# Fused attention and two MLPs on one core: the down-sampled attention units interleaved with the last local ones

## What is computed

```python
q_d = q.reshape(B, H, Sd, factor, D).mean(axis=3)      # factor 4: 576 -> 144 positions
k_d = k.reshape(B, H, Sd, factor, D).mean(axis=3)
v_d = v.reshape(B, H, Sd, factor, D).mean(axis=3)
out_up = np.repeat(sm_attn(q_d, k_d, v_d), factor, axis=2)
mask = np.abs(pos[:, None] - pos[None, :]) < factor     # local: 3 keys to either side
scores = np.where(mask, scale * np.matmul(q, k.transpose(0, 1, 3, 2)), -1000000000.0)
out_local = softmax(scores) @ v
x = out_up + out_local                                  # then (2304, 512)
x = (silu(rms_norm(x) @ w_gate) * (rms_norm(x) @ w_val)) @ w_out    # d_ff 1536
y = np.square(np.maximum(x @ w_in, 0)) @ w_out2                     # d_ff 2048
```

## Time and profile before

| | us |
|---|---|
| median of 3 runs (lowest, highest) | 1017.39 (1017.31, 1018.33) |
| the profiled execution, device time | 1024.89 |
| span of its trace | 1022.9 |

### The profile page before, as it was taken

The page is one execution under the profiler, slowest core; times in us unless marked ns, Lnnn a source line. Parts: engine busy times, 40 slices in busy tenths (PEclk is TensorE's granted clock), DMA queues, the critical chain, the costliest instruction groups (busy, mean ns, idle before and its releaser), DMA issues.

```text
span 1022.9 us, 16131 instructions
## 1 busy us (share of the span) xinstructions
PE 989.4 (97%) x6404; PEld 918.7 (90%) x6404; DVE 423.8 (41%) x783; ACT 322.0 (31%) x698; POOL 162.9 (16%) x151
## 2 busy tenths in 40 slices
PE   6899959999999999999999999999999999999998
PEld 5677748999999999999999999999999999999997
DVE  6678892543443443443442322323333233332322
ACT  3556554442122122122123333223222222232221
POOL 3356556640000000000002661000000000000000
PEclk9779878999999999999999999999999999999999
DMA  9968302310000000000002440000000000000000
GB/s 241 175 149 211 89 2 93 123 53 1 1 1 1 1 1 1 1 1 1 1 1 64 133 133 2 1 1 32 1 31 1 1 31 1 16 16 1 31 1 31
DMA packets 27972, 42.84 MB, mean 42 GB/s; under 512 B 2300, under 2 KB 14972, under 8 KB 27516
## 3 DMA queue, kind: packets, MB, share of 16 engines
q1 hardware_dynamic: 26316, 40.64, 14.7%
q10 hardware_dynamic: 1584, 1.18, 0.4%
HBM read 37.10 MB, written 4.72 MB: 41 GB/s over the span
## 4 chain that ended last, share of the span: by engine, by line
PE 90%; DVE 5%; issue 3%; DMA 1%; ACT 1%; POOL 1%; SPq 0%; DVEq 0%; ACTq 0%
PE bank L986 49%; PE bank L1085 20%; PE bank L1017 15%; PE bank L922 1%; PE bank L941 1%; PE bank L962 1%; PE bank L916 1%; DVE sml L683 1%; PE bank L937 1%; PE bank L973 1%; DVE mxl L662 1%; DMA kp<-k_dram 1%; DVE qd L705 1%; PE bank L911 0%; PE bank L885 0%
## 5 line engine op out<-in xcount | busy, mean ns | idle before, releaser
L986 PE MATMUL bank<-xs,wsplitB 128*128 128x384 f32 x2376 | 436.8, 335 | 0.0
L986 PEld LDWEIGHTS bank<-xs,wsplitB 128*128 128x128 f32 x2376 | 416.8, 188 | 6.9
L1085 PE MATMUL bank<-wsplitB 128*128 128x512 f32 x702 | 174.4, 393 | 0.0
L1085 PEld LDWEIGHTS bank<-wsplitB 128*128 128x128 f32 x702 | 130.7, 188 | 23.7
L840 DVE TENSOR_TENSOR prod<-sig 128x384 f32<-128x384 f32 x96 | 53.6, 558 | 222.2 <-ACT sig L605 222.2
L1017 PE MATMUL bank<-hb,wsplitB 128*128 128x384 f32 x720 | 136.1, 336 | 1.4 <-ACT hb L545 1.4
L1017 PEld LDWEIGHTS bank<-hb,wsplitB 128*128 128x128 f32 x720 | 125.6, 188 | 3.3 <-POOL wsplitB L419 1.6
L798 DVE TENSOR_TENSOR prod<-prod,bank 128x384 f32<-128x384 f32 x72 | 39.9, 554 | 192.5 <-PE bank L986 192.4
L605 ACT ACTIVATE sig<-bank 128x384 f32<-128x384 f32 x96 | 47.2, 492 | 229.5 <-PE bank L986 229.5
L545 ACT CAST hb<-prod 128x384 fp32r<-128x384 f32 x72 | 37.0, 514 | 248.1 <-DVE prod L798 248.1
L986 PE MATMUL bank<-xs,wsplitA 128*128 128x384 f32 x504 | 96.4, 343 | 3.8 <-DVE xs L766 3.8
(11 more groups left out here) (75 smaller groups left out, 746.4 us busy)
## 6 DMA issues: line engine op xcount, KB each, us to landing
wrawB<-w_dram SPq DMA_DIRECT2D x56, 256.0 KB, 3.0
vquad<-v_dram SPq DMA_DIRECT2D x16, 288.0 KB
out_dram<-work SPq DMA_DIRECT2D x18, 256.0 KB, 2.0
kp<-k_dram SPq DMA_DIRECT2D x3, 1152.0 KB, 13.7
qs<-q_dram SPq DMA_DIRECT2D x3, 1152.0 KB, 20.8
vwin<-v_dram SPq DMA_DIRECT2D x6, 512.0 KB
wrawA<-w_dram SPq DMA_DIRECT2D x12, 256.0 KB, 4.7
vwin<-v_dram SPq DMA_DIRECT2D x2, 320.0 KB
```

The costliest lines, as they stand in the source:

```text
L986: last = mm(bank[:, 0:cols], wslot(n)[:, pw, 128 * k:128 * k + 128], x[:, px, k, 0:cols], start=(i == 0 and k == 0), stop=(i == 2 and k == ...
L1085: last = mm(OUT[par][tt][:, :], gs[:, px, 128 * tt:128 * tt + 128], w[:, pw, :], start=(m == 0 and i == 0), stop=(m == J2 - 1 and i == 2))
```

## The change

The order of the units in a group becomes a string, `LLLLLLDLDLDLD` (L local, D down-sampled): six local units, then down-sampled and local ones in turn. The numbering helpers follow it. The lists of slots change with it, and so do three waits: each down-sampled unit waits only for the sums of four of its own pair of heads; the loads of the next groups wait for the last local unit, now at place 11 in the group and not at 8; the additions on GpSimd stand in four slots running.

```diff
+ORDER = "LLLLLLDLDLDLD"
+LAST_LOCAL = ORDER.rindex("L")
...
-SUM_FOUR_AT = (1, 3, 5, 7)
+SUM_FOUR_AT = (1, 2, 4, 5)
 FIRST_SUM_FOUR_AT = (4, 5, 6, 7)
-SUM_V_AT = (10, 11, 12)
-ADD_DOWN_AT = (5, 7, 11, 12)
+SUM_V_AT = (7, 8, 9)
+ADD_DOWN_AT = (5, 6, 7, 8)
...
         def local(g):
-            return g % NU < NL
+            return ORDER[g % NU] == "L"
...
-                    sp.wait_ge(qk_done, NU * (b - 2) + NL)
+                    sp.wait_ge(qk_done, NU * (b - 2) + LAST_LOCAL + 1)
...
-                    sp.wait_ge(pv_done, NU * (b - 2) + NL)
+                    sp.wait_ge(pv_done, NU * (b - 2) + LAST_LOCAL + 1)
...
-                if i == NL:
-                    pe.wait_ge(ks_done, 4 * (b + 1))
-                    if b == 0:
+                if not local(g):
+                    pe.wait_ge(ks_done, 4 * b + 2 * (i // 2) + 2)
+                    if b == 0 and i == 0:
                         pe.wait_ge(zeroed, 7)
```

More of the change, by code:

```diff
@@ L226, in local, with rank @@
         def local(g):
-            return g % NU < NL
+            return ORDER[g % NU] == "L"
+        def rank(g):
+            return ORDER[:g % NU].count(ORDER[g % NU])
         def nth(g):
-            b, i = g // NU, g % NU
-            return NL * b + i if i < NL else ND * b + i - NL
+            return (NL if local(g) else ND) * (g // NU) + rank(g)
         def unit(is_local, n):
-            return NU * (n // NL) + n % NL if is_local else NU * (n // ND) + NL + n % ND
+            count, kind = (NL, "L") if is_local else (ND, "D")
+            return NU * (n // count) + [i for i in range(NU) if ORDER[i] == kind][n % count]
         def first_turn(g):
             b, i = g // NU, g % NU
-            return NT * b + (i if i < NL else NL + 2 * (i - NL))
+            return NT * b + ORDER[:i].count("L") + 2 * ORDER[:i].count("D")
         def turns(g):
@@ L274, in down @@
         def down(g):
-            i = g % NU - NL
+            i = rank(g)
             return i // 2, i % 2
@@ L353, in _ @@
                 if n == PA:
-                    sp.wait_ge(qk_done, NU * (NG - 2) + NL)
-                    sp.wait_ge(pv_done, NU * (NG - 2) + NL)
+                    sp.wait_ge(qk_done, NU * (NG - 2) + LAST_LOCAL + 1)
+                    sp.wait_ge(pv_done, NU * (NG - 2) + LAST_LOCAL + 1)
                     sp.wait_ge(ks_done, 4 * (NG - 1))
@@ L479, in keep_output @@
                 act.wait_ge(pv_done, g + 1)
-                b, i = group_of(g), g % NU
+                b, i = group_of(g), rank(g)
                 if local(g):
@@ L489, in keep_output @@
                     ready(act, x_done, ND * b)
-                    nc.scalar.mul(outd[:, i - NL, :], output_bank(g)[:, 0:SD], 1.0 / FACTOR).then_inc(oe_done, 1)
+                    nc.scalar.mul(outd[:, i, :], output_bank(g)[:, 0:SD], 1.0 / FACTOR).then_inc(oe_done, 1)
             def split_high(n):
@@ L887, in qk @@
             def qk(g):
-                b, i = group_of(g), g % NU
-                if b == 0 and i in (0, 2):
+                b, i = group_of(g), rank(g)
+                if local(g) and b == 0 and i in (0, 2):
                     pe.wait_ge(k_part[i // 2], 16)
                     pe.wait_ge(q_part[i // 2], 16)
-                if (b == 0 and i == 5) or (b > 0 and i == 0):
+                if local(g) and i == (5 if b == 0 else 0):
                     pe.wait_ge(k_in[b], 16)
                     pe.wait_ge(q_in[b], 16)
-                if i == 0 and b < 2:
+                if local(g) and i == 0 and b < 2:
                     pe.wait_ge(zeroed, 3 * b + 3)
-                if i == NL:
-                    pe.wait_ge(ks_done, 4 * (b + 1))
-                    if b == 0:
+                if not local(g):
+                    pe.wait_ge(ks_done, 4 * b + 2 * (i // 2) + 2)
+                    if b == 0 and i == 0:
                         pe.wait_ge(zeroed, 7)
@@ L945, in values @@
             def values(g):
-                b, i, n = group_of(g), g % NU, nth(g)
+                b, i, n = group_of(g), rank(g), nth(g)
                 pe.wait_ge(te_done, first_turn(g) + turns(g))
```

## The result

The changed kernel takes 1028.3 us (median of 9 runs, 1022.76 to 1031.23) where the kernel before takes 1017.52 on the same chip (9 runs, 1016.34 to 1019.75). The ratio is 1.0102, with a 95% interval of 1.0080 to 1.0123: slower by 10.8 us, and outside the range that was forecast. The profiled execution of after took 1031.23, 2.9 above its median; that of before took 1024.89, 7.4 above its own. Between the two profiled executions the difference is 6.3 us.

What follows compares the result with a forecast made beforehand. Attention was taken as bound by loads (group 0), PE (groups 1, 2) and DVE (last group). Terms -3.05 (group 1) + 0.75 (group 2) + 0.8 (group 0) - 0.9 (last) = -2.4 us, from 1017.4 to 1015.0; range 1008.0 to 1020.5.

Steps and rivals of the forecast that it cites:

- The sum of work: PE's work in each attention group: 26.3 us at full clock before and after, no work added.
- The waits of a group: PE's waits for DVE and GpSimd in each group: 3.7 us in sum, between 0.5 and 5.5.
- The wait of slot 6: Group 0: PE waits 2.1 us for the sums of four (`qd`) before its first down-sampled scores.
- DVE and GpSimd meet: Within a group, one waits till the other's operation is through: 1.5 us added to PE's wait, bounds 0 and 3.7.
- The last group: Last attention group, bound by DVE: 0.9 us gained, between -1.5 and 2.
- The clock term: Every group: clock falls at about slot 10, 5 us low in place of 13.6, 2.2 us lost, bounds 0 and 6.0.
- the start of group 1: Group 1 starts at the low clock for some 3 us, 1.2 us lost, making it 33.7 us.
- Group 0: First attention group, behind the loads: 0.8 us lost, between -0.5 and +2.5; group 1 begins at 40.3.
- Carrying over the 7.5 us: Whole kernel: profiled 1024.89 lies 7.5 us above the median; difference carried over as it is, 1017.4 - 2.4 = 1015.0.
- The clock stays low longer: Rival: clock falls in every mixed stretch, 10 us low per group, new waits on top; +3.2, 1020.6 us, chance 0.20.
- The clock holds: Rival: local scores in every second slot keep 2.4 GHz through the waits; -8.6, 1008.8 us, chance 0.22.
- The loads bind: Rival: q and v of group 1 land 2 us later, so group 1 starts later; about 1017, no change, chance 0.13.

Runs made afterwards that it cites:

- e13: Changed kernel with filler matmuls in all groups, in PE's waits and behind down-sampled scores; 1020.87 us, ratio 1.0026 to the kernel before.
- r2: The kernel before, unedited, profiled a third time; its profiled execution was taken at 1016.95 us.
- e10: Kernel before with only group 0 mixed, from place 7 and not 6 on (additions of v in 8, 9, 10); 1023.73 us, ratio 1.0040.
- e12: As e2, with filler matmuls in group 0 where PE would wait; 1023.82 us, ratio 1.0054 to the kernel before.
- e2: Kernel before with the new order and places of side work in group 0 only; 1021.54 us, ratio 1.0046.

## Why the prediction was wrong

**The sum of work was right, and the waits in one group of two.** PE's work did not change (the rests above, 108.5 and 108.2). The waits of a group were forecast at 3.7 us, between 0.5 and 5.5, and idle time in groups 1 and 2 is 4.2 and 3.0. Only in group 2 are they the waits that were forecast (0.9 for `pd`, 0.8 for `prob`, 1.3 for `vd`). In group 1 the agreement is luck: of the 4.2 the pause makes 4.04. PE came to every other instruction without finding VectorE or GpSimd late, so the term was filled by something that it did not contain. The wait of slot 6 was forecast at 2.1 and is 2.62. DVE and GpSimd meet as the earlier trace rows had it (the normalisation at 62.02 took 1.88 against 0.91 alone). The last group gained 1.3, forecast 0.9. Group 1 did not wait for q.

**The clock term failed.** The forecast had 5 us low in a group and 2.2 us lost, and 1.2 more at the start of group 1, because every second slot has local scores and six local slots follow. The clock loss of groups 1 and 2 in after is 6.4 and 4.3 us, against 3.4 and 2.2. Of the three falls in the mixed stretches, one went as forecast (106.4, back after 6.8 us); after the other two the clock stayed low for 20.4 us, through local scores in every second slot, and after the second into the next group. The step took "it came back only once local scores had returned at 76.22" for a rule, from one case. What brought the falls was missed too: the one at 65.4 lies within the pause, which no term had, and not behind a forecast wait.

**Group 0 failed.** It was given 0.8 us, at most 2.5; it took 4.5. The step had the clock fall only "from the second wait on". It fell at the first, at 21.1, and the clock loss is 9.0 us against 2.7. That this alone made the group longer isn't shown: e13's group 0 took 43.7 us with the clock low for 6.8, a pause of 2.86 us and its filler in it.

**Carrying over the 7.5 us failed.** The sum was made against an execution of 1024.89 and the difference to the median carried over as it is. r2 shows what that hid: the gain of 3.05 us in group 1 was forecast against 36.75 us, a length that the median execution doesn't have (28.1 in r2). Against r2, even the forecast 33.7 and 32.5 of groups 1 and 2 would have been losses of 5.6 and 3.0 us. Of the miss of 13.2 us (+10.8 against -2.4), 8.7 is the sum's error on the profiled pair (+6.3 against -2.4), and 4.5 is this step.

**The rivals.** "The clock stays low longer" (1020.6, chance 0.20) named one part of the mechanism: some 15 us more at the low clock, at most 6 to 7 of the 10.8 us. It was too small by the same carried-over step and by group 0 (+2 against +4.5). "The clock holds" had 31 and 30.3 us for groups 1 and 2, and e13, where the clock holds in both, measured 31.9 and 30.4; but e13 has 40 filler matmuls in each of them, which the rival hadn't, so the agreement is partly luck. Even with the clock up the order is no faster than before, because the base was too slow. "The loads bind" was wrong as told; but the loads entered by another way, as they made PE's program come late. No rival had the pauses that follow from it, though the trace of before has them, 0.92 us at 61.41 and 1.31 at 98.97.

Two things are open. How the 4 us and more that don't come through the clock divide between waits and pauses no run tells. Nor why a mixed group 0 alone costs 4 to 6 us in the median even where its own length doesn't suffer (e10, e12): in the traces of e2, e10 and e12 the clock falls in group 1 with or behind a pause of 3.50, 1.32 and 2.80 us, but one trace each can't show that a mixed group 0 makes such pauses likelier or longer.

## What to carry to other kernels

When the times of a kernel spread more than the effect in question, the profiled execution must be placed among them before anything is costed against it: here a trace 7 us above the median showed a slow group that the median doesn't have, and a second trace near the median would have turned the sign of the sum. The granted clock of all the runs says more of the clock's share than any one trace. Mixing small matmuls of two kinds did not bring the clock back sooner: two of three falls in the mixed stretches lasted 20.4 us. A wait of PE that can't be removed and stands ahead of long dense work is worth filling with idle matmuls (2.9 us here); filler within attention gained 8 us in the new order and nothing in the old. Where a gap of PE is marked "issue", count the instructions ahead of it and look at the instruction queues of the profile: here every such gap was a wait for the next part of the program, and heavy loads made it late.

## What the hardware showed that was not expected

The clock stays at 1.2 GHz for as long as 20.5 us while PE is never idle (20.50 of 20.50 in r2 and in e10, and from 21.1 to 41.5 in after) and scores, transposes and values of attention run in it without a gap. The Trainium skill ("TensorE: Matmul & The Clock Gate", What's actually happening) says that the clock is released by a busy window; these stretches don't agree with that, if busy means that the profile shows matmuls back to back. With filler among the same matmuls, some 12 us of it, the clock loss fell from 23.6 to 4.4 us.

PE pauses in the middle of a row of like matmuls, 0.36 to 4.04 us at a time, where no operand can be waited for. All 39 such pauses of 0.3 us and more in the 19 traces came where 449 instructions of PE had begun, or 449 and a multiple of 256, and ended 1.35 to 1.78 us after a packet of 16384 bytes on the instruction queue q8 had landed; the DMA engines had a share of 0.93 to 1.12 while that packet had yet to start. In e10 one of 1.06 us, from 99.90 on, came at a DMA share of 0.02: the packet had been late before (98.30 to 99.61, after a share of 1.00). In after the clock fell within such a pause.
